# A one-core attention and mixer kernel: two fewer filler matmuls, the `u4` loads on another queue, and one semaphore step in place of two

## The chip, the cores and the metric

The kernel runs on one core of a Trainium2 chip. Its time is the device time of one execution in microseconds (us). It has five engines: TensorE (PE, with its weight loads shown apart as PEld), VectorE (DVE), ScalarE (ACT), GpSimd (POOL) and SyncE (SP), which issues DMAs.

## The reference

Attention with random features over 4 batches of 8 heads, 576 tokens and head size 64, then two mixers over the tokens and the channels:

```
def phi(x):                      # x: 576 x 64 of one head
    proj = x @ w_phi             # 128 features
    proj = proj - max(abs(proj)) # a maximum for each token
    return concat(exp(proj), exp(-proj))
kv, z = phi(k).T @ v, sum of phi(k) over the tokens
x = (phi(q) @ kv) / (phi(q) @ z + 1e-6)

u = x + (x.T @ U @ V).T          # U: 576 x 32, V: 32 x 576
x = u + relu(u @ w_ch1) @ w_ch2  # 512 -> 2048 -> 512
u = x + (relu(x.T @ w_tok1) @ w_tok2).T   # 576 -> 256 -> 576
out = u + relu(u @ w_ch1') @ w_ch2'       # 512 -> 1536 -> 512
```

## The kernel before

All products are taken in a short float format (fp32r) with a high and a low part: `a*b` is `a_hi*b_hi + a_hi*b_lo + a_lo*b_hi`, so that most matmuls come in threes. Heads are counted through: head `n` is head `n % 8` of batch `n // 8`. Two heads make a pair, `pn = n // 2`, since 2 times 64 channels fill the 128 partitions.

The program has three stages. In the **prologue** the 8 heads of batch 0 go through attention. In **block 1** PE works through the channel mixer in chunks of up to 512 tokens; woven into its matmuls, at places that tables of numbers give (`HEAD_STEPS`, `PAIR_STEPS`, `LAST_PAIR_STEPS`), are the attention steps of the 24 heads of batches 1 to 3. **Block 2** is the second mixer. Each engine has one instruction stream that runs in the order in which it is written, and waits on semaphores where its data come from another engine. Within a stream nothing overtakes a waiting instruction, but for weight loads.

Steps of one head: `proj_k` and `proj_qt` multiply the raw k and q (split into high and low part by `prep_k` and `prep_q` on ACT and POOL) by `w_phi`. `turn_r` turns q's block maxima on PE for the subtraction in `less_max`, `exp_k` and ACT's part of `less_max` take exponentials, `kv` builds the key-value product and `out` the head's output.

Three places matter here.

**The fillers.** `run_on_ones(count)` issues matmuls of ones whose result nobody reads. Each is two passes in the trace (a pass is one MATMUL record with its weight load). `WARM = 10, 5`: 10 at the start, and 5 ahead of `turn_r` of head 0, which waits for DVE's block maxima of q (`rq_done`).

**The loads of `u4`** (`U` of the first mixer, four copies side by side, 240 KB in six DMAs, whose contiguous pieces are 128 or 256 bytes of each partition and tile). They are issued from ACT's queue, two ahead of `kv` 0, two ahead of `exp_k` 1 and two ahead of `kv` 1. The first reader is PE's `pair_u` of head 1, which waits for all six (`u4_in`). SP's queue issues everything else that the prologue needs: for n = 2 to 8 the k of head n, its tail once more, the q of head n, the v of head n-1, and then one or two pieces of the mixer's weights (`load_w`). Some of these wait until POOL or PE has done with the buffer.

**The pairs.** For each of the 12 pairs of batches 1 to 3, PE turns the pair's output into token order (`pair_t`, L783), 5 tiles in the bank `ps_a`; ACT copies them, rounded, into XPH (`x_pair_hi`, L962 and L963). DVE then takes the remainders in two subtractions: L1157 for the first 4 tiles (into XPL, `x_pair_lo`), and L1159 for the fifth, which is only 64 tokens long and whose remainder is put on the upper 64 partitions of XPH's own fifth tile. Each subtraction raises `xl_done` by one. PE multiplies the high part by U in `pair_u` (L801, four matmuls) and the rest in `pair_l` (L808, five matmuls), with `less_max` of the next head (L727, two matmuls) between them for three pairs of four, and nothing between them for the last pair of a batch. `pair_l` waits for the first subtraction ahead of its first matmul and for the second ahead of its fifth.

Of the kernel before, what the change touches and what calls it, by code (L numbers as in the profile page):

```python
# [4 lines left out]
F32 = mybir.dt.float32  # L5
# [4 lines left out]
P = 128  # L10
B, H, S, DH = 4, 8, 576, 64
# [19 lines left out]
NB = S // TB  # L31
TURN = 72
WCH = 2 * D
WARM = 10, 5

K0 = 2 * P

# [292 lines left out]
def mixer_kernel(nc, k_t, q_t, v_aug, w_phi, u4, v4, mask_in, ident_in, wa, wb, wt1_in, wt2_in, x2_d, out):  # L330
# [181 lines left out]
    def wait(eng, name, value):  # L512
        if value > 0:
            eng.wait_ge(sem[name], value)
# [34 lines left out]
    def _(sp):  # L549
# [34 lines left out]
        for n in range(2, H + 1):  # L584
            load_k(n)
            load_k_again(n)
            load_q(n)
            load_v(n - 1)
            for i in ((n - 2,) if n < 6 else (2 * n - 8, 2 * n - 7)):
                load_w(i)  # L590
        load_v(H)
        for i in range(2 * H - 6, 4 * G1):
            load_w(i)
# [58 lines left out]
    def _(pe):  # L652
# [5 lines left out]
        def ring_free(use):  # L658
            if use >= AFTER:
                if use < AFTER + WIDE - RING:  # L660
                    pe.wait_ge(sem["x_done"], B * H)
                    pe.wait_ge(sem["xt_copied"], B * DT)
                    pe.wait_ge(sem["xl_done"], 2 * (B - 1) * DT)
                    pe.wait_ge(sem["kvl_done"], (B - 1) * H)
                    pe.wait_ge(sem["xu_lo"], B * DT)
                pe.wait_ge(sem["ring_read"], use - WIDE + 1)
            elif use >= RING:
                pe.wait_ge(sem["ring_read"], use - RING + 1)
            elif use < 2:
                pe.wait_ge(sem["qp_done"], 2 * (H - 1))  # L670
            else:
                pe.wait_ge(sem["x_done"], H)

        def turned_read(pairs):
            wait(pe, "xt_copied", pairs)
            wait(pe, "xl_done", 2 * (pairs - DT))

        def step(name, n, first=False):
            pn = n // 2
# [75 lines left out]
            elif name == "out":  # L755
                wait(pe, "tsum_done", 2 * (before(("proj_k",), (name, n)) - H) - 1)
                turned_read(before(("pair_t",), (name, n)))
                wait(pe, "x_done", n)
                wait(pe, "qp_done", 2 * n + 2)
                wait(pe, "kvl_done", steady(n))  # L760
                for a in range(2):
                    for c in range(2):
                        cols = slice(c * CW, (c + 1) * CW)
                        pe.matmul(x_ps[:, c, :], KVH[:, a, :], QPH[:, a, cols], start=(a == 0), stop=False)  # L764
                        pe.matmul(x_ps[:, c, :], KVL[:, a, :], QPH[:, a, cols], start=False, stop=False)  # L765
                for a in range(2):
                    pe.wait_ge(sem["qpl_done"], 2 * steady(n) - 1 + a)
                    for c in range(2):
                        cols = slice(c * CW, (c + 1) * CW)
                        last = pe.matmul(x_ps[:, c, :], KVH[:, a, :], QPL[:, a, cols], start=False, stop=(a == 1))  # L770
                last.then_inc(sem["out_done"], 1)
            elif name == "pair_t" and first:
                wait(pe, "x_done", n + 1)
                wait(pe, "diff_done", before(("proj_k",), (name, n)))
                for t in range(ST):
                    last = pe.transpose(xt_banks[:, t * P:(t + 1) * P], XP[:, t, :], ID[:])
                last.then_inc(sem["xt_done"], 1)
            elif name == "pair_t":
                wait(pe, "x_done", n + 1)
                wait(pe, "tsum_done", 2 * (before(("proj_k",), (name, n)) - H) - 1)  # L780
                for t in range(ST):
                    k = min(P, S - t * P)
                    last = pe.transpose(xt_banks[0:k, t * P:(t + 1) * P], UT[:, pn % DT, t * P:t * P + k], ID[:])  # L783
                last.then_inc(sem["xt_done"], 1)
            elif name == "pair_u":
                if first:
                    wait(pe, "x_done", n + 1)
                    wait(pe, "kv_copied", before(("kv",), (name, n)))
                    if n == 1:
                        pe.wait_ge(sem["u4_in"], loaded(6))  # L790
                    for t in range(ST):
                        last = pe.matmul(xu_bank(n), U4[:, t, :], XP[:, t, :], start=(t == 0), stop=(t == ST - 1))
                    last.then_inc(sem["xu_done"], 1)
                else:
                    wait(pe, "xt_copied", pn + 1)
                    wait(pe, "kvl_done", before(("kv",), (name, n)) - H)
                    wait(pe, "tsum_done", 2 * (before(("proj_k",), (name, n)) - H))
                    if pn == DT:
                        pe.wait_ge(sem["u_split"], 2)
                    for t in range(FULL):  # L800
                        pe.matmul(xu_bank(n)[0:2 * RANK], U2[:, t, 0:2 * RANK], XPH[:, t, :], start=(t == 0), stop=False)  # L801
            elif name == "pair_l":
                pe.wait_ge(sem["xl_done"], 2 * (pn - DT) + 1)
                for t in range(ST):
                    if t == FULL:
                        pe.wait_ge(sem["xl_done"], 2 * (pn - DT) + 2)
                    x = XPL[:, t] if t < FULL else XPH[:, FULL]
                    last = pe.matmul(xu_bank(n)[0:2 * RANK], U2[:, t, 0:2 * RANK], x, start=False, stop=(t == ST - 1))  # L808
                last.then_inc(sem["xu_done"], 1)
# [97 lines left out]
    def _(act):  # L907
# [90 lines left out]

        act.dma_start(WPR[0:DH, :], w_phi).then_inc(sem["wphi_in"], 16)
        act.dma_start(RAW[0:DH, S:SP], k_t[0, 0][:, FULL * P:S]).then_inc(sem["rk_again_0"], 16)  # L1000
        def load_u4(rows, tiles, source):
            for cols in (slice(0, RANK), slice(2 * RANK, P)):
                act.dma_start(U4[rows, tiles, cols], u4[source, tiles, cols]).then_inc(sem["u4_in"], 16)

        for name, n in PROLOGUE["act"]:
            if (name, n) == ("kv", 0):
                load_u4(slice(0, P), slice(0, FULL), slice(0, P))
            if (name, n) == ("exp_k", 1):
                load_u4(HALF[0], FULL, HALF[0])
            if (name, n) == ("kv", 1):  # L1010
                load_u4(HALF[1], FULL, HALF[0])
            if (name, n) == ("prep_q", 1):
                act.wait_ge(sem["ident_in"], loaded(1))
                act.copy(SPREAD[0:TB], ID[0:TB, 0:NB]).then_inc(sem["spread"], 1)
# [54 lines left out]
    def _(dve):  # L1069
        def step(name, n, first=False):  # L1070
# [83 lines left out]
            elif name == "pair_t" and not first:  # L1154
                dve.wait_ge(sem["kp_done"], 2 * before_on_dve(("proj_k",), (name, n)))
                dve.wait_ge(sem["xt_copied"], pn + 1)
                dve.tensor_tensor(XPL[:, 0:FULL].rearrange("p t f -> p (t f)"), xt_banks[:, 0:FULL * P],  # L1157
                                  XPH[:, 0:FULL].rearrange("p t f -> p (t f)").bitcast(F32), ALU.subtract).then_inc(sem["xl_done"], 1)
                dve.tensor_tensor(XPH[HALF[1], FULL], xt_banks[0:S_LAST, FULL * P:], XPH[0:S_LAST, FULL].bitcast(F32),  # L1159
                                  ALU.subtract).then_inc(sem["xl_done"], 1)  # L1160
            elif name == "pair_u":
# [259 lines left out]
```

## Time and profile before

| | us |
|---|---|
| median of 3 runs | 959.62 (959.57 to 959.8) |
| the profiled execution | 959.57 |
| its span, first to last instruction | 957.6 |
| PE busy in it | 953.1 |
| DVE, ACT, POOL busy | 510.1, 373.7, 238.1 |

What lies around the span, 959.57 - 957.6, is 2.0 us. Times within a trace are given as us from the span's start. Busy time of PE is the union of its records; a matmul's record is longer than the distance to the next one, since matmuls are pipelined.

### The profile page before, as it was taken

The page shows a single profiled execution, that of the slowest core. Times are in us where ns is not written, and L with a number is a line of the kernel's source. Part 1 is how long each engine was busy: PE and PEld are TensorE (multiplying, and loading weights), DVE is VectorE, ACT ScalarE, POOL GpSimd, SP SyncE. Part 2 cuts the span into 40 slices and gives each one's busy share as a digit, 9 for nine tenths or more (in the row PEclk, how much of TensorE's full clock was granted, in tenths as well). Part 3 has the DMA queues.
Part 4 walks back from the last instruction along what each step waited for, and adds up shares of the span by engine and source line. Part 5 has one row for each costly group of instructions (what it writes and reads, how often), then busy time and mean ns, then how long its engine had stood idle before and what let it go on. Part 6 is the DMA issues. An engine that isn't in the chain of part 4 may idle for free.

```text
span 957.6 us, 14160 instructions
## 1 busy us (share of the span) xinstructions
PE 953.1 (100%) x5402; PEld 830.3 (87%) x5402; DVE 510.1 (53%) x1005; ACT 373.7 (39%) x795; POOL 238.1 (25%) x148
## 2 busy tenths in 40 slices
PE   9999999999999999999999999999999999999998
PEld 8998888888888888888888889988888888888898
DVE  6756777667777658778543333433443343343232
ACT  6757667626665445665321112321212211111111
POOL 4357566704344214442120003430000000000000
PEclk9999999999999999999999999999999999999999
DMA  7661111111111021110052005542142132010010
GB/s 197 178 205 29 45 31 36 44 44 44 33 35 44 22 66 26 41 44 9 18 178 83 23 1 176 182 111 65 50 116 83 50 94 94 12 44 1 1 44 23
DMA packets 43042, 62.75 MB, mean 66 GB/s; under 512 B 10656, under 2 KB 30304, under 8 KB 41952
## 3 DMA queue, kind: packets, MB, share of 16 engines
q1 hardware_dynamic: 33376, 52.35, 18.7%
q10 hardware_dynamic: 9600, 9.50, 3.1%
q8 instruction: 44, 0.72, 0.3%
q14 instruction: 22, 0.18, 0.1%
HBM read 47.68 MB, written 14.16 MB: 65 GB/s over the span
## 4 chain that ended last, share of the span: by engine, by line
PE 98%; DVE 1%; DMA 0%; ACT 0%; issue 0%; ACTq 0%; DVEq 0%
PE ps_ring L872 50%; PE ps_a L872 15%; PE ps_m L872 8%; PE ps_m L743 6%; PE ps_ring L752 2%; PE ps_t L714 2%; PE ps_a L770 1%; PE ps_a L765 1%; PE ps_a L764 1%; PE ps_a L705 1%; PE ps_t L727 1%; PE ps_a L695 1%; PE ps_m L738 1%; PE ps_t L654 1%; PE ps_t L656 1%; PE ps_t L655 1%
## 5 line engine op out<-in xcount | busy, mean ns | idle before, releaser
L872 PE MATMUL ps_ring<-u_hi,w_hi 128*128 128x512 f32 (+1 forms) x376 | 143.6, 382 | 0.1
L872 PE MATMUL ps_ring<-h_hi,w_hi 128*128 128x512 f32 (+1 forms) x376 | 143.0, 380 | 0.1
L872 PE MATMUL ps_ring<-u_hi,w_lo 128*128 128x512 f32 (+1 forms) x376 | 141.1, 375 | 0.0
L872 PE MATMUL ps_ring<-u_lo,w_hi 128*128 128x512 f32 (+1 forms) x376 | 141.0, 375 | 0.0
L872 PE MATMUL ps_ring<-h_lo,w_hi 128*128 128x512 f32 (+1 forms) x376 | 140.8, 374 | 0.0
L872 PE MATMUL ps_ring<-h_hi,w_lo 128*128 128x512 f32 (+1 forms) x376 | 140.6, 374 | 0.0
L1035 ACT ACTIVATE h_hi<-ps_ring 128x512 fp32r<-128x512 f32 (+1 forms) x94 | 53.1, 565 | 174.2 <-PE ps_ring L872 173.4
L1262 DVE SCALAR_TENSOR_TENSOR h_lo<-ps_ring,h_hi 128x512 fp32r<-128x512 f32 (+1 forms) x94 | 60.8, 648 | 106.1 <-ACT h_hi L1035 105.9
L1327 POOL TENSOR_TENSOR q_features_lo<-q_features_t,q_features_hi 128x576 fp32r<-128x576 f32 x48 | 67.8, 1433 | 115.7 <-ACT q_features_t L954 115.7
L1345 POOL TENSOR_TENSOR w_lo<-w_raw,w_hi 128x1024 fp32r<-128x1024 f32 x28 | 67.5, 2427 | 116.5 <-ACT w_hi L985 115.3
L872 PEld LDWEIGHTS ps_ring<-h_lo,w_hi 128*128 128x128 f32 x376 | 70.8, 188 | 13.3 <-DVE h_lo L1262 0.2
L872 PEld LDWEIGHTS ps_ring<-u_hi,w_lo 128*128 128x128 f32 x376 | 70.8, 188 | 13.2
L872 PEld LDWEIGHTS ps_ring<-u_hi,w_hi 128*128 128x128 f32 x376 | 70.9, 189 | 12.0 <-DVE h_lo L1262 0.5
L872 PEld LDWEIGHTS ps_ring<-h_hi,w_hi 128*128 128x128 f32 x376 | 71.0, 189 | 11.2 <-DVE acc L1197 0.5
L872 PEld LDWEIGHTS ps_ring<-u_lo,w_hi 128*128 128x128 f32 x376 | 71.0, 189 | 9.6
L872 PEld LDWEIGHTS ps_ring<-h_hi,w_lo 128*128 128x128 f32 x376 | 71.0, 189 | 9.4
L1197 DVE TENSOR_TENSOR acc<-ps_ring,acc 128x512 f32<-128x512 f32 (+1 forms) x67 | 43.3, 647 | 56.9 <-PE ps_ring L872 56.6
L1338 POOL TENSOR_TENSOR q_split<-kq_raw,q_split 64x640 fp32r<-64x640 f32 x27 | 41.8, 1550 | 62.0 <-ACT q_split L923 54.8
L1333 POOL TENSOR_TENSOR k_split<-kq_raw,k_split 64x640 fp32r<-64x640 f32 x27 | 42.2, 1563 | 57.2 <-ACT k_split L919 52.7
L743 PE MATMUL ps_m<-v_one,k_features 128*128 128x66 f32 x448 | 53.1, 272 | 0.0
L743 PEld LDWEIGHTS ps_m<-v_one,k_features 128*128 128x128 f32 x448 | 52.2, 192 | 0.0
L1035 ACT ACTIVATE h_hi<-ps_a 128x512 fp32r<-128x512 f32 (+1 forms) x30 | 15.8, 526 | 84.5 <-PE ps_a L872 84.0
(218 smaller groups left out, 1951.2 us busy)
## 6 DMA issues: line engine op xcount, KB each, us to landing
w_raw<-in_wa SPq DMA_DIRECT2D x16, 512.0 KB, 5.1
w_raw<-in_wb SPq DMA_DIRECT2D x12, 512.0 KB, 4.2
v_one<-in_v_aug SPq DMA_DIRECT2D x28, 165.0 KB, 2.2
x_features<-x_scratch SPq DMA_DIRECT2D x4, 1152.0 KB, 6.1
x_by_tokens<-x_turned SPq DMA_DIRECT2D x16, 288.0 KB, 5.3
u_full<-x_scratch SPq DMA_DIRECT2D x4, 1152.0 KB, 5.2
kq_raw<-in_q_t SPq DMA_DIRECT2D x28, 160.0 KB, 2.9
x_tokens<-x_by_tokens SPq DMA_DIRECT2D x16, 256.0 KB, 2.7
```

Source lines behind the costliest of these rows:

```text
L654: pe.matmul(ps, wh, xh, start=first, stop=False)
L714: last = pe.matmul(turned_ps(n)[:, c, :], WP[:, i, :], sq(n)[:, c * CW:(c + 1) * CW], start=(i == 0), stop=(i == 1))
L743: last = pe.matmul(kv_ps[:, a, :], kp(n)[:, 2 * t + a], v(n)[:, t, :], start=False, stop=(a == 1 and t == FULL - 1))
L752: last = pe.matmul(out_bank[0:k, t, :], QP[:, a, t * P:t * P + k], KV[:, a, 0:VC], start=(a == 0), stop=(a == 1))
L872: last = pe.matmul(ps, w, x, start=(k, m) == (0, 0), stop=ended)
L1035: act.activation(HH[:, j, 0:n], bank(use, n), ACT.Relu).then_inc(sem["h_hi"], 1)
L1197: dve.tensor_tensor(ACC[:, j, 0:n], ps, ACC[:, j, 0:n], ALU.add).then_inc(sem["ring_read"], 1)
L1262: dve.scalar_tensor_tensor(out=HL[:, j, 0:n], in0=bank(USE[block_no, c, u], n), scalar=0.0, in1=HH[:, j, 0:n].bitcast(F32), op0=ALU.max, o ...
L1327: pool.tensor_tensor(QPL[:, a, 0:S], QP[:, a, 0:S], QPH[:, a, :].bitcast(F32), ALU.subtract).then_inc(sem["qpl_done"], 1)
L1333: pool.tensor_tensor(sk(n)[DH:P, :], raw_kq(n)[0:DH, :], sk(n)[0:DH, :].bitcast(F32), ALU.subtract).then_inc(sem["k_split_lo"], 1)
L1338: pool.tensor_tensor(sq(n)[0:DH, :], raw_kq(n)[DH:P, :], sq(n)[DH:P, :].bitcast(F32), ALU.subtract).then_inc(sem["q_split_lo"], 1)
L1345: pool.tensor_tensor(WL[place], WR[place], WH[place].bitcast(F32), ALU.subtract).then_inc(sem["w_lo"], 1)
```

## The change

It has three parts. Two of the five fillers ahead of `turn_r` 0 go. The six `u4` loads leave ACT's queue and are issued from SP's, one after another, behind the first piece of the mixer's weights and ahead of the k of head 3; their shapes are the same, their order differs a little. And `xl_done` is raised once for a pair, by the second subtraction, so that all five matmuls of `pair_l` come after one wait for it; the counts of the other waits on `xl_done` are halved to match.

```diff
-WARM = 10, 5
+WARM = 10, 3
...
             for i in ((n - 2,) if n < 6 else (2 * n - 8, 2 * n - 7)):
                 load_w(i)
+            if n == 2:
+                for cols in (slice(0, RANK), slice(2 * RANK, P)):
+                    sp.dma_start(U4[:, 0:FULL, cols], u4[:, 0:FULL, cols]).then_inc(sem["u4_in"], 16)
+                    for rows in HALF:
+                        sp.dma_start(U4[rows, FULL, cols], u4[HALF[0], FULL, cols]).then_inc(sem["u4_in"], 16)
...
-                    pe.wait_ge(sem["xl_done"], 2 * (B - 1) * DT)
+                    pe.wait_ge(sem["xl_done"], (B - 1) * DT)
...
-            wait(pe, "xl_done", 2 * (pairs - DT))
+            wait(pe, "xl_done", pairs - DT)
...
-                pe.wait_ge(sem["xl_done"], 2 * (pn - DT) + 1)
+                pe.wait_ge(sem["xl_done"], pn - DT + 1)
                 for t in range(ST):
-                    if t == FULL:
-                        pe.wait_ge(sem["xl_done"], 2 * (pn - DT) + 2)
...
-        def load_u4(rows, tiles, source):
-            for cols in (slice(0, RANK), slice(2 * RANK, P)):
-                act.dma_start(U4[rows, tiles, cols], u4[source, tiles, cols]).then_inc(sem["u4_in"], 16)
-
         for name, n in PROLOGUE["act"]:
-            if (name, n) == ("kv", 0):
-                load_u4(slice(0, P), slice(0, FULL), slice(0, P))
-            if (name, n) == ("exp_k", 1):
-                load_u4(HALF[0], FULL, HALF[0])
-            if (name, n) == ("kv", 1):
-                load_u4(HALF[1], FULL, HALF[0])
...
                 dve.tensor_tensor(XPL[:, 0:FULL].rearrange("p t f -> p (t f)"), xt_banks[:, 0:FULL * P],
-                                  XPH[:, 0:FULL].rearrange("p t f -> p (t f)").bitcast(F32), ALU.subtract).then_inc(sem["xl_done"], 1)
+                                  XPH[:, 0:FULL].rearrange("p t f -> p (t f)").bitcast(F32), ALU.subtract)
```

On PE, the end of a pair in block 1, with each row's waits. Before:

```order
L727 MATMUL ps_t<-q_max_rows,minus_ones 128x288
L808 MATMUL ps_m<-x_pair_lo,u_split 64x128 [waits xl_done]
L808 MATMUL ps_m<-x_pair_lo,u_split 64x128 x3
L808 MATMUL ps_m<-x_pair_hi,u_split 64x128 [waits xl_done]
L872 MATMUL ps_ring<-h_hi,w_hi 128x512 [waits h_hi,w_lo,ring_read]
```

and after the change, with the new line numbers:

```order
L732 MATMUL ps_t<-q_max_rows,minus_ones 128x288
L811 MATMUL ps_m<-x_pair_lo,u_split 64x128 [waits xl_done]
L811 MATMUL ps_m<-x_pair_lo,u_split 64x128 x3
L811 MATMUL ps_m<-x_pair_hi,u_split 64x128
L875 MATMUL ps_ring<-h_hi,w_hi 128x512 [waits h_hi,w_lo,ring_read]
```

No matmul moves; the fifth one's wait is gone, and the first one's now stands for both subtractions.

On SP's queue, between the first piece of weights and the k of head 3 (`u_82` is `u4`):

```order
@@ -14,4 +14,8 @@
 L568 DMA v_one_odd<-in_v_aug 64x66
 L574 DMA w_raw<-in_wa 128x1024
+L593 DMA u_82<-in_u 128x4x32
+L595 DMA u_82<-in_u 64x32 x2
+L593 DMA u_82<-in_u 128x4x64
+L595 DMA u_82<-in_u 64x64 x2
 L553 DMA kq_raw_odd<-in_k_t 64x576
 L557 DMA kq_raw_odd<-in_k_t 64x64
```

Six DMAs are put in; all that stood behind them keeps its order.

## Rows read from the trace of the kernel before

**Rows 1.** The page: busy us of each engine; PE's granted clock in 40 slices.
```profile
PE 953.1 (100%) x5402; PEld 830.3 (87%) x5402; DVE 510.1 (53%) x1005; ACT 373.7 (39%) x795; POOL 238.1 (25%) x148
...
PEclk9999999999999999999999999999999999999999
```

**Rows 2.** Waits of PE: us in total, times, longest us.
```profile
PE ps_t L727 <- DVE q_max_rows L1119: 0.2, 1, 0.2
```

**Rows 3.** Timeline, an ordinary pair: start us, us, engine, line, count.
```profile
114.45 0.69 DVE L1157 TENSOR_TENSOR x_pair_lo<-ps_a,x_pair_hi 128x512 fp32r<-128x512 f32 x1 [0.44 <-ACT x_pair_hi L963]
...
115.03 0.48 PE L727 MATMUL ps_t<-q_max_rows,minus_ones 128*128 128x288 f32 x2
115.17 0.28 DVE L1159 TENSOR_TENSOR x_pair_hi<-ps_a,x_pair_hi 64x128 fp32r<-64x128 f32 x1
...
115.35 0.40 PE L808 MATMUL ps_m<-x_pair_lo,u_split 128*64 128x128 f32 x4
...
115.59 0.23 PE L808 MATMUL ps_m<-x_pair_hi,u_split 128*64 128x128 f32 x1
...
115.65 0.44 PE L872 MATMUL ps_ring<-h_hi,w_hi 128*128 128x512 f32 x1
```

**Rows 4.** Timeline, the last pair of a batch.
```profile
198.33 0.28 DVE L1159 TENSOR_TENSOR x_pair_hi<-ps_a,x_pair_hi 64x128 fp32r<-64x128 f32 x1
...
198.36 0.45 PE L808 MATMUL ps_m<-x_pair_lo,u_split 128*64 128x128 f32 x4
198.67 0.27 PE L808 MATMUL ps_m<-x_pair_hi,u_split 128*64 128x128 f32 x1
198.78 0.45 PE L872 MATMUL ps_ring<-h_hi,w_hi 128*128 128x512 f32 x1
```

**Rows 5.** Line L1159: count, ns min/median/max, first and last start us.
```profile
L1159 DVE TENSOR_TENSOR x_pair_hi<-ps_a,x_pair_hi x12: 283/283/285, 115.2 to 467.2; 64x128 fp32r<-64x128 f32 x12
```

**Rows 6.** Timeline of DVE, two neighbours that each raise a semaphore.
```profile
78.15 1.23 DVE L1097 TENSOR_REDUCE k_proj_sum<-ps_a 128x512 f32<-128x1024 f32 x1 [0.34 <-PE ps_m L705]
79.29 0.41 DVE L1098 TENSOR_REDUCE k_proj_sum<-ps_m 128x128 f32<-128x256 f32 x1
```

**Rows 7.** Timeline of PE at the start: the fillers and `turn_r` 0.
```profile
1.00 4.53 PE L879 MATMUL ps_m<-k_features_odd 128*64 128x128 f32 x20 [1.00 <-POOL k_features_odd L1310]
...
7.84 1.31 PE L879 MATMUL ps_m<-k_features_odd 128*64 128x128 f32 x10
9.53 0.28 PE L722 MATMUL ps_ring<-ident,q_block_max 128*72 128x128 f32 x1 [0.39 <-DVE q_block_max L1106]
```

**Rows 8.** Timeline of SP's queue: issues of the first weights, k 3, q 3, v 3.
```profile
8.98 0.59 SPq L574 DMA_DIRECT2D w_raw<-in_wa  x1
9.80 0.47 SPq L553 DMA_DIRECT2D kq_raw_odd<-in_k_t  x1
...
11.41 0.47 SPq L562 DMA_DIRECT2D kq_raw_odd<-in_q_t  x1
...
18.43 0.33 SPq L567 DMA_DIRECT2D v_one_odd<-in_v_aug  x1
```

**Rows 9.** Tile `u`: the issues on ACT's queue, ns min/median/max.
```profile
L1003 ACTq DMA_DIRECT2D u<-in_u x6: 389/516/837, 11.1 to 16.5; - x6
```

**Rows 10.** Timeline of ACT: the splits of q 3 and k 3, `kv` 1, `less_max` 1.
```profile
16.60 0.72 ACT L923 CAST q_split_odd<-kq_raw_odd 64x640 fp32r<-64x640 f32 x1
17.35 0.72 ACT L919 CAST k_split_odd<-kq_raw_odd 64x640 fp32r<-64x640 f32 x1
18.43 0.27 ACT L944 COPY v_k<-ps_m 128x132 f32<-128x132 f32 x1 [0.36 <-PE ps_m L743]
19.19 1.19 ACT L954 ACTIVATE q_features_t<-ps_t 128x576 f32<-128x576 f32 x2 [0.48 <-PE ps_t L727]
```

**Rows 11.** DMA issues, KB each, us to landing: q 3's alone, and the page's median.
```profile
kq_raw_odd<-in_q_t SPq DMA_DIRECT2D x1, 160.0 KB, 4.5
```
```profile
kq_raw<-in_q_t SPq DMA_DIRECT2D x28, 160.0 KB, 2.9
```

## Prediction, written before the run

> **What bounds the kernel now.** I read the page first, for which engine has no idle time; then the waits of PE, for whether anything makes it wait; then the timelines of the three places that the change touches, row by row, because none of them is large enough to show in a sum.
>
> The page says that PE is busy for 953.1 of 957.6 us and DVE for 510.1 [rows 1]. So PE is the bound, and not on average only: among the waits that the trace lists, the only one of PE behind the first 10 us is 0.2 us for DVE's `q_max_rows` [rows 2]. It follows that **every tenth that PE loses anywhere is lost at the end**, and that what other engines gain is worth nothing unless PE waits for it. But the list has a blind spot. Two matmuls that start a little late because of a semaphore still look busy, since a record is longer than the step to the next. One has to look at the distances between starts, and that is where the largest term of this change lies.
>
> **Part 1, the pairs (12 times).** Nothing is taken from PE's work. What changes is what its first of five matmuls waits for: the second subtraction (L1159) rather than the first (L1157). There are 12 such places, all alike [rows 5].
>
> *Ordinary pair (9 of 12)* [rows 3]. The first subtraction ends at 114.45 + 0.69 = 115.14. PE starts the first of the five at 115.35, behind `less_max`, the fifth at 115.59 and the mixer's next matmul at 115.65. The second subtraction ends at 115.17 + 0.28 = 115.45. So before the change, PE began the four matmuls while DVE was still at the fifth tile, and the fifth came just when that was ready. Afterwards all five start behind 115.45.
>
> How long from DVE's end to PE's start? The last pair of a batch shows that [rows 4]: L1159 ends at 198.33 + 0.28 = 198.61, the matmul that waits for it starts at 198.67, 0.06 later. And what do five matmuls take from a standing start? There too: the group of four has records that last 0.45 together, against 0.40 in a running stream [rows 3], so standing costs 0.05 more. In the running stream the fifth follows the first by 115.59 - 115.35 = 0.24; from a standing start I take 0.24 + 0.05 = 0.29 to 0.30.
>
> Ordinary pair after the change: start at 115.45 + 0.06 = 115.51, fifth at 115.51 + 0.30 = 115.81, next matmul one step of 0.06 later, 115.87, against 115.65: **+0.22**.
>
> *Last pair of a batch (3 of 12)* [rows 4]. The fifth is held by the second subtraction already, at 198.67, and the next matmul follows at 198.78. After: first at 198.67, fifth at 198.97, next at 199.03: **+0.25**.
>
> Sum: 9 x 0.22 + 3 x 0.25 = 1.98 + 0.75 = **2.7 us**. Behind it no work is idle enough to give this back: PE is in no debt to anyone that a later slack could repay [rows 1, 2], and each of the others gets its input from PE later by the same amount. Bounds: at the low end the standing start costs nothing (fifth 0.24 behind the first), 9 x 0.16 + 3 x 0.19 = 2.0; at the high end each place costs what the fifth was ahead of in a last pair, the whole of 198.67 - 198.36 = 0.31, so 12 x 0.31 = 3.7.
>
> The missing step of the semaphore might help DVE: would L1159 start earlier if L1157 raised nothing? L1159 starts 0.03 behind L1157's end [rows 3]. The neighbours L1097 and L1098 do overlap: 78.15 + 1.23 = 79.38, but L1098 starts at 79.29, 0.09 before, and L1097 does raise a semaphore [rows 6]. So raising one is not what keeps L1159 back, and taking it away should not let it go earlier. I put 0 here; as a rival it is priced below.
>
> The Trainium skill has a rule on just this (VectorE: DVE Perf Modes, "Two Vector instructions with no wait between them"): an instruction whose output starts in another group of 32 partitions than the last output is held until all earlier ones are done, and a semaphore operation plays no part in it. L1159 writes the upper half where L1157 wrote from partition 0. By that rule part 1 costs the 2.7 us; without it, were L1159 free to overlap, it would be the 1.4 us of the first rival.
>
> **Part 2, the fillers.** The five fillers are ten records in 1.31 us, from 7.84 to 9.15; `turn_r` 0 starts at 9.53, released by DVE after PE had been idle for 0.39 [rows 7]. Two fewer are four records, 4 x 0.131 = 0.52 us, which only lengthen that idle time to some 0.9 us. Time saved: 0, since DVE's block maxima are what is late. The fillers hide nothing but the quiet of PE, and what that quiet may cost is its clock. The granted clock reads full in every slice [rows 1], but the pace of the fillers tells more: 4.53 / 20 = 0.227 us a record for the first ones, 0.131 for the later ones [rows 7], so the first ran at 1.2 GHz and the later ones at 2.4. A fall back would double the duration of what follows. I take 0, because PE is quiet for 0.4 us already without any slowing behind it, and 0.9 is closer to that than to nothing at all having run; the other end is in the rivals.
>
> **Part 3, the `u4` loads.** ACT loses six issues of 0.39 to 0.84 us [rows 9]. They are issued by its sequencer beside running work, and ACT's steps around them are released by PE [rows 10]: no gain. SP gets them between the end of the first weights' issue, 8.98 + 0.59 = 9.57, and k 3 [rows 8]. At six times the median of 0.52 that is 3.1, with small gaps 3.3 us: k 3 is issued at about 12.9 rather than 9.80, q 3 some 1.1 us later, at 14.0 rather than 11.41. Behind them v 2, the next weights, k 4 and q 4 move too, by less and less, until v 3, which waits for PE until 18.43 in any case [rows 8]; from there on SP is as before.
>
> Who misses k 3 and q 3? ACT, in order: it splits q 3 at 16.60, k 3 at 17.35, then copies `kv` 1 and takes `less_max` 1 at 19.19, for which PE waits [rows 10]. From the start of q 3's split to the earliest `less_max` it is 0.75 + 0.75 + 0.30 = 1.8 us, so q 3 may land as late as 19.19 - 1.8 = 17.4 at no cost. Landing took 4.5 us there, in a stretch crowded by weights, and 2.9 in the median [rows 11]. The two ends are 14.0 + 2.9 = 16.9, cost 0, and 14.0 + 4.5 = 18.5, cost 18.5 - 17.4 = 1.1 us of PE. In between: before, q 3 landed at 11.41 + 4.5 = 15.9 with much of `u4` still on its way, and now all of `u4` goes ahead of it in the same queue. Its 240 KB are 1.5 times q 3's 160 KB, in small pieces; a delay of 1.5 us or so gives 17.4, right at the edge. I take **0.1 us**.
>
> **Sum.** 2.7 + 0 + 0.1 = 2.8 us. The profiled execution would take 959.57 + 2.8 = 962.4 (a span of 957.6 + 2.8 = 960.4), and since it lies 0.05 from the median of 959.62, the median too: **962.4 us**.
>
> **Rivals.**
>
> *DVE starts its second subtraction earlier (not slower).* One mechanism at one place: if it is the raised semaphore after all that separates L1157 and L1159, then L1159 moves from 0.03 behind to 0.08 or 0.09 before L1157's end, as L1098 does [rows 6], 0.11 earlier. If the five matmuls also cost nothing extra from a standing start, a pair costs 0.16 - 0.11 = 0.05 and a last pair 0.19 - 0.11 = 0.08, in all 0.7 us; with the extra, 9 x 0.11 + 3 x 0.14 = 1.4 us, and 0.1 for part 3. The time is 960.3 to 961.1, of which I take 961.0, close to the end that keeps the extra. It decides from 0.16 us a pair downwards: 12 x 0.16 is the 1.9 us below which a measurement would call it no change. For it: both instructions work on different tiles and nothing in the code makes the second wait. Against: the pair in [rows 6] overlaps with its semaphore.
>
> *The pairs cost nothing.* The starts of modelled records are not exact, and the first four matmuls may already come so late in truth that the fifth's wait is the same wait. Then the time is 959.6 to 960.0. Against it: all 12 places read alike [rows 5], and starts, unlike ends, are recorded.
>
> *ACT misses q 3.* The upper end of part 3, 1.1 us of PE lost near 19, on top of the 2.7: 959.6 + 2.7 + 1.1 = 963.4. For it: that stretch of SP's queue is full.
>
> *PE's clock falls in the longer quiet ahead of `turn_r` 0.* Then the PE work behind 9.53 runs at half pace for some us; each us of it costs another, 2 to 3 us at the rate of the first fillers [rows 7]. Time: 964.4 to 965.4. Against it: the remaining fillers still stand ahead of it.
>
> *Faster.* It would take a gain that no row offers: the fillers and ACT's issues are both in time that nobody waits for. I leave 0.02 for a mechanism that I can't name.
>
> **How the numbers follow.** Chances: the forecast (a loss of 2.0 to 3.4 us) 0.70; DVE earlier 0.11; no cost 0.06; ACT misses q 3 0.08; clock 0.03; faster 0.02. A measurement of this kernel tells a change from none at about 0.2%, 1.9 us, so slower begins at 961.5. Slower: 0.70 + 0.08 + 0.03, less a little for forecasts at their low end, 0.80. Within 0.2%: 0.11 + 0.06 + that little, 0.18. Faster: 0.02. The range goes down to the first rival's time, 961.0, and up to 963.9, over the upper bound of part 1 (959.6 + 3.7 + 0.1 = 963.4) and the third rival. What is left out is no cost, the clock, faster, and the lower half of the first rival, some 0.16.
>
> **What would show it.** In the timeline after the change, in each of the 12 places all five matmuls of `pair_l` start behind the end of the second subtraction, the first 0.06 later; the mixer's next matmul follows the second subtraction's end by 0.42 (115.87 - 115.45) rather than 0.20. If that distance is 0.3, the standing start is cheap; if the second subtraction starts before the first one ends, the first rival holds. The trace's waits of PE should now list this line, which they did not. For part 3: k 3 issued at about 12.9, and `less_max` 1 on ACT at 19.2 if the slack held. For part 2: `turn_r` 0 at 9.53 as before, and then the same pace. I would be wrong above all if the distances between starts in [rows 3, 4] are an artefact, since all of 2.7 us rests on them.

## The result, and the profile after

The change makes the kernel slower: 966.29 us in the median of four executions (965.09 to 968.15), against 959.66 for the kernel before on the same chip (959.57 to 959.8). The ratio is 1.007, with an interval of 1.0051 to 1.009. The prediction was 962.4 us with a range of 961.0 to 963.9: right in its sign, too low by 3.9 us, and the time lies above the range.

The profiled execution of the changed kernel took 961.59 us (span 959.6), which would have fitted the forecast. It is not typical, and that is the first finding. Its granted clock was 1.000; the four others had spans of 963.0 to 966.1 us and mean granted clocks of 0.995 to 0.996. A mean of 0.996 over 963.0 us means 0.004 x 963.0 = 3.9 us of clock missing, 0.995 over 966.1 us means 4.8; the third digit is rounded, so each is good to 0.5. The kernel before had 1.000 in every execution whose clock is listed. So two questions stand: where did the 2.0 us of the profiled execution go, and what takes PE's clock in the others?

The waits of PE after the change, where before there was one entry behind the first 10 us [rows 2] (engine, tile and line that wait, the releaser; us in total, times, longest us):

```profile
PE ps_ring L727 <- DVE q_block_max L1099: 0.8, 1, 0.8
PE ps_m L743 <- ACT k_features L938: 0.7, 1, 0.7
PE ps_m L811 <- DVE x_pair_hi L1152: 0.6, 3, 0.3
...
PE ps_t L732 <- DVE q_max_rows L1112: 0.2, 1, 0.2
```

The third is the pairs, which the prediction asked for. The first is the quiet that the missing fillers leave, also foreseen. The second is new, and the prediction has nothing on it: PE's `kv` 2 waits for ACT's `k_features`. Of the twelve pairs this list of PE shows three. The list of the weight loads (PEld) shows all of them:

```profile
PEld ps_m L811 <- DVE x_pair_hi L1152: 3.0, 12, 0.4
```

**The pairs.** Timeline of the changed kernel, all engines, the ordinary pair that answers to [rows 3] (start us, us, engine, line, count):

```profile
115.14 0.69 DVE L1150 TENSOR_TENSOR x_pair_lo<-ps_a,x_pair_hi 128x512 fp32r<-128x512 f32 x1 [0.44 <-ACT x_pair_hi L966]
...
115.84 0.28 DVE L1152 TENSOR_TENSOR x_pair_hi<-ps_a,x_pair_hi 64x128 fp32r<-64x128 f32 x1
...
116.18 0.46 PE L811 MATMUL ps_m<-x_pair_lo,u_split 128*64 128x128 f32 x4
...
116.48 0.22 PE L811 MATMUL ps_m<-x_pair_hi,u_split 128*64 128x128 f32 x1
...
116.54 0.44 PE L875 MATMUL ps_ring<-h_hi,w_hi 128*128 128x512 f32 x1
```

DVE ends at 115.84 + 0.28 = 116.12, the first matmul starts 0.06 behind it, the fifth 0.30 behind the first, and the mixer 0.06 behind the fifth: 0.42 from DVE's end to the mixer, as forecast, against 0.20 before.

**The start.** Timeline of PE (the last number in square brackets is its idle time before the row, and who ended it):

```profile
7.68 0.87 PE L882 MATMUL ps_m<-k_features_odd 128*64 128x128 f32 x6
9.38 0.28 PE L727 MATMUL ps_ring<-ident,q_block_max 128*72 128x128 f32 x1 [0.84 <-DVE q_block_max L1099]
```

The three fillers end at 7.68 + 0.87 = 8.55 and `turn_r` 0 follows when DVE has its maxima. This whole trace lies 0.15 us earlier than that of before [rows 7], and PE had been idle for 0.84 instead of 0.39.

**The loads.** Timeline of the changed kernel, SP's queue, ACT and PE, which answers to [rows 8] and [rows 10]:

```profile
9.46 0.44 SPq L593 DMA_DIRECT2D u<-in_u  x1
...
11.78 1.15 SPq L595 DMA_DIRECT2D u<-in_u  x2
...
12.98 0.60 SPq L553 DMA_DIRECT2D kq_raw_odd<-in_k_t  x1
...
14.27 0.59 SPq L562 DMA_DIRECT2D kq_raw_odd<-in_q_t  x1
...
17.19 1.64 SPq L557 DMA_DIRECT2D kq_raw<-in_k_t  x1
17.34 0.72 ACT L926 CAST q_split_odd<-kq_raw_odd 64x640 fp32r<-64x640 f32 x1 [0.91 <-DMA kq_raw_odd<-in_q_t]
...
19.04 1.19 ACT L957 ACTIVATE q_features_t<-ps_t 128x576 f32<-128x576 f32 x2
...
22.01 0.72 ACT L922 CAST k_split<-kq_raw 64x640 fp32r<-64x640 f32 x1 [1.78 <-DMA kq_raw<-in_k_t]
...
23.70 0.46 PE L743 MATMUL ps_m<-v_one,k_features 128*128 128x132 f32 x2 [0.70 <-ACT k_features L938]
```

And the same view of the kernel before, of the stretch that the prediction did not look at:

```profile
14.40 0.60 SPq L557 DMA_DIRECT2D kq_raw<-in_k_t  x1
...
20.30 0.73 ACT L919 CAST k_split<-kq_raw 64x640 fp32r<-64x640 f32 x1
...
21.97 0.40 ACT L929 ACTIVATE k_features<-k_proj_less_max_first,sign 128x128 f32<-128x128 f32 x1 [0.95 <-DVE k_proj_less_max_first L1090]
...
23.04 0.46 PE L738 MATMUL ps_m<-v_one,k_features 128*128 128x132 f32 x2
```

Read the two together. k 3 and q 3 move as forecast (12.98 and 14.27 for a forecast of 12.9 and 14.0), ACT takes `less_max` 1 at 19.04: q 3 costs nothing. But behind them k 4 moves by nearly as much: its second piece is issued at 17.19 rather than 14.40. ACT splits k 4 just ahead of the exponentials of `exp_k` 2, in order. Before, that split started at 20.30 and could have started 0.95 later, since `exp_k` 2 waited that long for DVE. Now the data lets ACT start only at 22.01, `exp_k` 2 follows, and PE starts `kv` 2 at 23.70 instead of 23.04.

The account of the profiled execution: at the mixer's first matmul, at 62.27 before and 62.93 after, the changed kernel is 0.66 us behind; the twelve pairs add 0.17 to 0.24 each, some 2.4; about 1.1 of that is given back in between (the fourth experiment shows where); it ends 2.02 behind.

### The profile page after: what moved, and what is told of

It is laid out like the page before. It is cut to its first block, busy times and chain, and to the rows that moved or that the text cites. A ratio compares the mean times of both kernels' runs of the same rounds, so it can differ in the third digit from the quotient of the medians.

```text
span 959.6 us, 14152 instructions
## 1 busy us (share of the span) xinstructions
PE 953.0 (99%) x5398; PEld 828.7 (86%) x5398; DVE 510.3 (53%) x1005; ACT 373.4 (39%) x795; POOL 238.1 (25%) x148
## 4 chain that ended last, share of the span: by engine, by line
PE 97%; SPq 1%; DMA 1%; DVE 1%; issue 0%; ACT 0%; ACTq 0%; DVEq 0%
PE ps_ring L875 50%; PE ps_a L875 15%; PE ps_m L875 8%; PE ps_m L748 5%; PE ps_t L719 2%; PE ps_ring L757 1%; PE ps_a L775 1%; PE ps_a L770 1%; PE ps_a L769 1%; PE ps_a L710 1%; PE ps_t L732 1%; PE ps_t L661 1%; PE ps_t L660 1%; PE ps_t L659 1%; PE ps_m L743 1%; PE ps_a L788 1%
```

## The experiments

All are the kernel before with one edit, except the fifth and the last. "Before" was timed beside each, at 959.59 to 959.85 us.

**1. Three fillers instead of five.**

```
-WARM = 10, 5
+WARM = 10, 3
```

> The kernel before with WARM = 10, 3 and nothing else. Theory A (the two fillers cost the clock): most executions 963 to 966 us, with a mean granted clock of 0.995 to 0.996 in them, while an execution that happens to keep full clock takes 959.5. Theory B (the clock is lost only where several longer quiet stretches of PE come together, so not by the fillers alone): 959.6, clock 1.000 throughout. Theory C (the clock has nothing to do with the fillers): 959.6 as well.

Measured: 959.61 us (959.21 to 960.0, 10 executions), ratio 0.9998, interval 0.9989 to 1.0008, the clock 1.000 in all. Part 2 costs nothing, though PE waits 0.8 us for `turn_r` 0.

**2. No fillers ahead of `turn_r` 0.**

```
-WARM = 10, 5
+WARM = 10, 0
```

> The kernel before with WARM = 10, 0, so that PE is quiet for about 1.7 us ahead of turn_r 0. Theory A: at least as slow as with 3 fillers, 963 to 968, and the profile should show where the clock is low: matmul steps of 0.11 us twice as far apart in the stretch behind 9.5 us, or the slow pace of the first fillers lasting longer. Theories B and C: 959.6, since nothing waits for the fillers.

Measured: 974.68 us (974.39 to 975.05, 4 executions), ratio 1.0153, interval 1.0138 to 1.0168, the clock 0.982 in all. In its trace PE is idle for 1.9 us ahead of `turn_r` 0, where with five fillers it was 0.39. Its windows (stretch us; busy time of PE, PEld, DVE, ACT and POOL with counts; PE's granted clock; DMA share; GB/s):

```profile
8.00:10.00 2.00, 0.45 (x2) 0.35 (x3) 1.41 (x2) 1.25 (x3) 1.93 (x2) 0.83 0.91 275
10.00:12.00 2.00, 2.00 (x11) 2.00 (x11) 1.41 (x4) 0.81 (x2) 1.93 (x2) 0.50 0.84 219
...
42.00:44.00 2.00, 2.00 (x14) 2.00 (x14) 0.85 (x3) 0.80 (x3) 0.39 (x1) 0.63 0.05 6
44.00:46.00 2.00, 2.00 (x20) 1.86 (x20) 1.29 (x3) 1.53 (x3) 0.37 (x1) 1.00 0.04 12
```

The clock falls to 0.50, its lower level of 1.2 GHz, in the quiet ahead of `turn_r` 0, and stays there for some 34 us (9.3 to 43.5) although PE is busy all the time: 11 matmuls in 2 us where there were 19. The fillers do hold the clock, and a fall costs far more than the quiet that brings it.

**3. The `u4` loads alone.** The six issues stand on SP where the change puts them; the rest is as before.

```
+            if n == 2:
+                for cols in (slice(0, RANK), slice(2 * RANK, P)):
+                    sp.dma_start(U4[:, 0:FULL, cols], u4[:, 0:FULL, cols]).then_inc(sem["u4_in"], 16)
...
-            if (name, n) == ("kv", 0):
-                load_u4(slice(0, P), slice(0, FULL), slice(0, P))
...
```

> The kernel before with only the u4 loads moved to SP's queue ahead of k 3. From the profile of the changed kernel: exp_k 2 on ACT comes late behind the split of k 4, PE waits 0.7 us at kv 2, in all +0.6 to +0.8: 960.3, clock 1.000. If the extra 0.7 us of quiet is what costs the clock (theory B or C): above 963 in most executions.

Measured: 965.22 us (963.64 to 965.84, 4 executions), ratio 1.0053, interval 1.0036 to 1.007, clocks of 0.994 to 0.996. So the part that was costed at 0.1 us brings most of the loss. Its profiled execution (964.74 us) fell into the typical case. The wait of PE:

```profile
PE ps_m L743 <- ACT k_features L940: 1.5, 1, 1.5
```

And its windows:

```profile
22.00:24.00 2.00, 1.52 (x14) 1.19 (x12) 1.41 (x4) 0.67 (x2) 0.16 (x1) 1.00 1.05 300
24.00:26.00 2.00, 0.97 (x9) 1.01 (x10) 1.75 (x6) 1.40 (x4) 1.54 (x1) 1.00 0.55 118
26.00:28.00 2.00, 2.00 (x16) 2.00 (x16) 0.00 (x0) 0.48 (x2) 0.00 (x0) 0.79 0.01 3
28.00:30.00 2.00, 2.00 (x11) 2.00 (x11) 0.18 (x1) 1.12 (x3) 0.00 (x0) 0.50 0.75 150
...
32.00:34.00 2.00, 2.00 (x12) 2.00 (x11) 0.85 (x3) 0.98 (x3) 0.20 (x1) 0.51 0.17 33
34.00:36.00 2.00, 2.00 (x19) 1.86 (x19) 0.96 (x3) 1.34 (x3) 0.56 (x1) 1.00 0.00 0
```

Here is the mechanism. PE, busy without a gap from 20 on, is quiet between 23.5 and 25.0 because `kv` 2 waits. Behind that the clock goes to half, from about 27.1 to 34, and PE works through that stretch at 11 matmuls in 2 us. The missing clock is, window by window, 2 x 0.21 + 2 x 0.50 + 2 x 0.50 + 2 x 0.49 = 3.4 us. `kv` 2 itself started at 25.02, which is 2.0 later than before. Together that is 5.4, and the execution is 964.74 - 959.57 = 5.2 longer.

In the changed kernel's own profile the wait was shorter, 0.70, and the clock held:

```profile
22.00:24.00 2.00, 1.29 (x12) 1.00 (x11) 1.34 (x5) 1.99 (x4) 1.24 (x2) 1.00 0.78 266
24.00:26.00 2.00, 2.00 (x20) 2.00 (x19) 1.29 (x4) 0.14 (x2) 0.34 (x1) 1.00 0.62 142
```

**4. The pairs alone.** One raise of `xl_done` behind the second subtraction, as in the change.

```
-                pe.wait_ge(sem["xl_done"], 2 * (pn - DT) + 1)
+                pe.wait_ge(sem["xl_done"], pn - DT + 1)
                 for t in range(ST):
-                    if t == FULL:
-                        pe.wait_ge(sem["xl_done"], 2 * (pn - DT) + 2)
...
```

> The kernel before with only the one xl_done step per pair. By the steps in the trace of the changed kernel: 12 places of +0.20 = +2.4, of which about 1.1 comes back at short waits of PE further on that the delay hides, so +1.3: 960.9 to 961.0. By the prediction as written (nothing comes back): 962.3. If the clock were lost here: above 963.

Measured: 961.11 us (960.48 to 962.13, 10 executions), ratio 1.0012, interval 1.0003 to 1.0022: 1.4 us, half of the 2.7 forecast. In its trace, as in that of the whole change, each of the 12 pairs puts PE back by about 0.2, and some 1.1 us comes back between them, a little at a time. Two places show how, in the kernel before and in the whole change. The first is the loads of `proj_k`'s weights, before and after (PEld: start us, us, count, idle before):

```profile
173.75 0.53 PEld L705 LDWEIGHTS ps_a<-w_phi_split,k_split 128*128 128x128 f32 x4 [0.37 <-issue]
```
```profile
174.84 0.53 PEld L710 LDWEIGHTS ps_a<-w_phi_split,k_split 128*128 128x128 f32 x4 [0.20 <-issue]
```

PE is busy in both, yet the loader stood still for 0.37 before and stands for 0.20 now; the mixer's next matmul is 0.17 less late behind it. The second, before the change:

```profile
333.08 0.19 PEld L872 LDWEIGHTS ps_ring<-h_hi,w_hi 128*128 128x128 f32 x1 [0.51 <-DVE acc L1197]
```

and the same load after the change:

```profile
334.72 0.19 PEld L875 LDWEIGHTS ps_ring<-h_hi,w_hi 128*128 128x128 f32 x1 [0.27 <-DVE acc L1190]
```

This load waits for DVE's `acc` both times, but for 0.27 instead of 0.51: the matmul ahead of it is 1.87 late, the load itself 1.64, and 0.24 come back. Most of these stops are at the loads for `proj_k`, of which the list of waits of the kernel before says:

```profile
PEld ps_a L705 <- issue: 2.4, 9, 0.4
```

After the change it is 1.9 for the same nine. That these short stops are slack is shown by the difference of the starts; what ends those that read `issue` was not tested.

**5. The whole change with five fillers.**

```
-WARM = 10, 3
+WARM = 10, 5
```

> The whole change, but with WARM = 10, 5 as before. Theory D (the loss is the late k 4, which makes PE wait at kv 2 and then costs it the clock, plus the pairs; the fillers do nothing): 965 to 967, clock 0.995 to 0.996, as the whole change. If the missing fillers lengthen or bring on the slow clock when the other parts are there: back to about 961.6, clock 1.000.

Measured: 966.82 us in the median of six executions, ratio 1.0063, interval 1.0043 to 1.0083 (both without the longest one). One had a clock of 1.000 and took 961.9; four took 965.23 to 968.3 at 0.995 and 0.996; one took 978.45 at 0.983. The two fillers make no difference to the whole change either. The profiled one (967.6 us) has the wait at `kv` 2 at 1.9 us and the clock at 0.50 from 25.4 to 35.7, which is 5.1 us of missing clock. It is the only trace of the three parts together in which the clock fell: `kv` 2 starts at 25.00, 2.0 later than before, and 2.0 + 5.1 + 1.4 for the pairs is 8.5, for a measured 965.6 - 957.6 = 8.0 of span. The four slower executions of the changed kernel itself have no trace; that their clock fell at the same place is concluded from this one and the third experiment.

**6. Six tiny DMAs on SP, `u4` still on ACT.** Each brings 32 bytes a partition into a tile that nobody reads.

```
+            if n == 2:
+                for j in range(6):
+                    sp.dma_start(TINY[:, 8 * j:8 * j + 8], mask_in).then_inc(sem["tiny_in"], 16)
```

> The kernel before, u4 still loaded from ACT's queue, and in addition six tiny DMAs (128 x 8 numbers each, into a tile nobody reads) on SP's queue at the place where the change puts the u4 loads. Theory D1 (what delays k 4 is that SP is kept busy issuing, some 3.3 us): PE waits 0.7 to 1.5 us at kv 2, 964 to 966 with a clock below 1. Theory D2 (it is the u4 bytes in small pieces, ahead of k 3 to k 4 in one queue): 959.6 to 960.0, clock 1.000.

Measured: 960.32 us (959.94 to 966.06, 10 executions), ratio 1.0015, interval 1.0 to 1.0029. Eight lie at 959.94 to 960.78 with the clock at 1.000; two took 964.21 and 966.06, at 0.996 and 0.995. The profiled one, of the first kind:

```profile
9.52 3.04 SPq L594 DMA_DIRECT2D tiny<-in_mask  x6
...
16.18 0.47 SPq L554 DMA_DIRECT2D kq_raw<-in_k_t  x1
...
22.14 0.72 ACT L923 CAST k_split<-kq_raw 64x640 fp32r<-64x640 f32 x1 [1.26 <-DMA kq_raw<-in_k_t]
```

The 3.0 us of issuing by themselves bring k 4's split from 20.30 to 22.14 and `kv` 2 from 23.04 to 23.83, with a wait of PE of 0.2 there. In the whole change the split was at 22.01, in the third experiment at 23.33. So against the third experiment SP's issue time is the larger part of the delay, 1.8 of 3.0 us. Where the clock fell in the two slower executions no trace shows. The fall is usual in the third experiment and rare here, so the rest of the delay matters too. That this rest comes from the bytes of `u4` ahead of k 4 is argued and not shown: the profiled execution of the whole change has those bytes, and its split is no later than here.

**7. The `u4` loads on SP, behind q 4.** The same six issues with `if n == 4`, between `load_q(4)` and `load_v(3)`.

```
             load_q(n)
+            if n == 4:
+                for cols in (slice(0, RANK), slice(2 * RANK, P)):
...
             load_v(n - 1)
```

> The kernel before with only the u4 loads moved to SP's queue, but behind q 4, ahead of v 3, where SP waits for PE in any case. Theory D: k 4 and q 4 are untouched, so no wait at kv 2; SP is some 1 us late afterwards and v 3 has slack: 959.6, clock 1.000. If moving the u4 loads off ACT's queue is itself what costs (their bytes, or their landing before pair_u of head 1): over 962.

Measured: 959.58 us (959.27 to 960.11, 10 executions), ratio 0.9999, interval 0.9989 to 1.0008, the clock 1.000 in all. The move from ACT to SP by itself costs nothing; what costs is the place of the loads, ahead of k 3 and k 4.

**8. Two fillers.**

```
-WARM = 10, 5
+WARM = 10, 2
```

> The kernel before with WARM = 10, 2: PE is quiet for about 1.1 us ahead of turn_r 0. With 3 fillers and 0.8 us nothing was lost, with none and 1.55 us the clock was low from 9 to 43 us. If the length of that quiet decides step by step: about 959.6 in most executions, a few at 965 or more. If the number of fillers hardly matters until the last are gone: 959.6 throughout.

Measured: seven of ten executions took 959.37 to 960.92 us at 1.000, three 972.96 to 973.23 at 0.984; median 959.96, ratio 1.0043, interval 1.0001 to 1.0084. The profiled one is of the first kind, and the fall did not come in it, though PE waited longer than with three fillers:

```profile
PE ps_ring L722 <- DVE q_block_max L1106: 1.2, 1, 1.2
```

So the same program, at the same place, keeps its clock in one execution and loses it in another.

**9. The third experiment with twenty fillers ahead of `kv` 2.** This separates the quiet from the lateness, since k 4 is as late as before.

```
                 wait(pe, f"v_in_{n % 2}", loaded(2 * (n // 2 + 1)))
+                if n == 2:
+                    WPS = WP[:, 0]
+                    for _ in range(20):
+                        pe.matmul(ps_m[:, 0:DF], WPS, WPS, start=True, stop=True)
```

> The kernel before, with the six u4 loads on SP at n == 2 as in e3_u4_sp, and 20 filler matmuls (128x128, some 0.06 us each, 1.2 us) on PE ahead of kv 2, between its wait for v and its wait for the k features. They fill most of the quiet that the late k 4 makes there (1.5 us in e3_u4_sp) and take nothing away from its lateness. Theory A (the lateness costs PE some 1 to 2 us, and the rest of e3_u4_sp's 5.5 us is PE's clock, which falls because PE is quiet at that place): the granted clock is 1.000 in all executions, and the time 960.6 to 961.8 us. Theory B (the clock falls for something else that the move does near 20 to 26 us, the transfers for instance, whatever PE does there): the clock is .994 to .996 as in e3_u4_sp and the time 964 to 966. Theory C (the lateness itself costs PE more than the wait shows, and the clock is a small part): clock 1.000, time 963 or more.

Measured: 961.61 us (961.37 to 962.59, 9 executions), ratio 1.0023, interval 1.0012 to 1.0033; the clock is 1.000 in eight and 0.998 in one. Timeline of PE and ACT, and the windows:

```profile
22.96 2.43 PE L745 MATMUL ps_m<-w_phi_split 128*128 128x128 f32 x20
23.09 0.73 ACT L928 CAST k_split<-kq_raw 64x640 fp32r<-64x640 f32 x1 [2.64 <-DMA kq_raw<-in_k_t]
...
25.23 0.44 PE L747 MATMUL ps_m<-v_one,k_features 128*128 128x132 f32 x2
```
```profile
24.00:26.00 2.00, 2.00 (x20) 2.00 (x20) 1.50 (x4) 1.16 (x3) 1.45 (x1) 1.00 0.95 245
26.00:28.00 2.00, 2.00 (x20) 2.00 (x19) 0.00 (x0) 0.51 (x2) 0.00 (x0) 1.00 0.07 19
```

`kv` 2 starts at 25.23, 2.2 later than before and even 0.2 later than in the third experiment, the same loads are issued in the same order, and yet the kernel is 3.6 us faster than that one, 961.61 against 965.22, because PE was not quiet. The 2.0 us that remain over before are the lateness of `kv` 2. Theory A holds, and B and C fall. (The fillers took 0.12 us each, not the 0.06 expected, and so were a little too long: they, and no longer the features, release `kv` 2. By the 0.75 us from the start of ACT's exponentials over 128x512 (24.27) to `kv` 2 in the third experiment, here 24.03 + 0.75 = 24.8, they hold it for about 0.4 us, an estimate.)

**10. The whole change with the `u4` loads behind q 4.**

```
-            if n == 2:
+            if n == 4:
```

(with the block moved up between `load_q(n)` and `load_v(n - 1)`, as in the seventh).

> The whole change, but with the u4 loads on SP behind q 4 (n == 4) rather than ahead of k 3, as in e7_u4_late. Theory A (of the change's 6.6 us the place of the u4 loads is all but the pairs' part, and the fillers are nothing): the pairs' 1.4 us alone are left, 960.8 to 961.4, clock 1.000, and no wait of PE at kv 2. Theory D (the three parts add up to more than each alone, for instance since fewer fillers and a later start of the pairs together leave PE more quiet near its limits): 963 or more, or a clock below 1 in several executions.

Measured: 961.13 us in the median. Nine of ten executions took 960.66 to 962.57 at 1.000, one took 974.8 at 0.984; ratio 1.0032, interval 1.0004 to 1.006. The median is 1.5 over before: the pairs' part and nothing else. The one outlier has the clock and the time of the outliers of the eighth experiment. Such a long fall came in none of the ten executions with three fillers alone, but it may also be what the 978.45 us of the fifth experiment are, with a clock of 0.983 and all five fillers. So it is rare rather than tied to the two fillers, and what brings it is open.

No version came out faster than the kernel before by more than the noise: each of the three parts costs something or nothing.

## Why the prediction was wrong, step by step

**What bounds the kernel: right.** "Every tenth that PE loses anywhere is lost at the end" held for `kv` 2, with one exception below.

**Part 1, the pairs: the mechanism right, its sum twice too large.** The distances came out as worked out: 0.06 from DVE to PE, 0.30 over the five matmuls, 0.17 to 0.24 a pair. The rival of an earlier second subtraction fell: it starts 0.70 behind the first (115.84 - 115.14), against 0.72 before [rows 3]. That is 0.02 nearer, at all twelve places, and not the 0.11 of the rival, and nothing overlaps. By the Trainium skill's rule that the prediction quoted (VectorE: DVE Perf Modes, "Two Vector instructions with no wait between them") the second subtraction is held with or without a semaphore, and the trace agrees with its 0.70. The step that failed is "behind it no work is idle enough to give this back". It was read off the list of waits, in which PE matmuls that keep busy have none; yet the weight loads in front of them stand still for up to 0.51 us at some places (the list of PEld's waits has nine stops of up to 0.4 at `proj_k` alone), and a PE that comes late there catches up. The 12 delays of about 0.20, some 2.4 in all, become 1.4 us, as the fourth experiment has it, instead of 2.7. The prediction itself had warned that this list has a blind spot, and applied that to the loss only.

**Part 2, the fillers: right.** Zero, by the first and the fifth experiment. The rival that the clock falls there was real as a mechanism (second and eighth experiments, with fewer fillers than the change leaves) but was sized wrongly: it gave 2 to 3 us of loss for a fall that takes 13 to 15, since the half clock lasts for some 34 us (second) rather than "some us". Its reading of the first fillers' pace holds: in the trace of the fourth experiment ten filler records at a granted clock of 0.50 take 2.40 us, 0.24 each, so 0.227 each at the start is near the lower level, though the view lists 1.00 there.

**Part 3, the `u4` loads: this is where the prediction failed.** The term "I take 0.1 us" measured 5.5 us by itself (third experiment, 965.22 against 959.72). The prediction looked at q 3, found the slack held at the edge, and wrote that k 4 and q 4 "move too, by less and less, until v 3". k 4's second piece moved by 2.8 us (14.40 to 17.19), not less than k 3's first by much (3.2). Who needs k 4 was never asked. The method that it used for q 3 would have shown the danger: k 4's split at 20.30 had 0.95 of slack, and the landings of the kernel before between 9 and 20 us list its second piece (KB, us to landing):

```profile
kq_raw<-in_k_t SPq DMA_DIRECT2D x1, 16.0 KB, 5.6
```

With the issue time measured after the change, 17.19 + 5.6 = 22.8 against 20.30 + 0.95 = 21.25: 1.5 us late. The runs show `kv` 2 late by 0.7 (whole change, profiled), 2.0 (third, and fifth) and 2.2 (ninth, some 0.4 of it from its fillers).

On the same step the Trainium skill says (DMA: Bandwidth & Descriptors, "Issuing engines are not separate DMA queues") that issuing from several engines saves only the sequencer's time to start a DMA, usually small beside the DMA. Here the six issues took 3.5 us in a row on SP (9.46 to 12.93), and in the sixth experiment 3.0 us of issuing alone put k 4's split back by 1.8: in a queue whose next entries are due, that time is not small.

**The clock: a rival at the wrong place.** It stood ahead of `turn_r` 0 with a chance of 0.03. The place is `kv` 2, where before the change PE had no quiet at all. The prediction costed a wait at its own length; a wait in this part of the kernel costs its length and, in most executions, the half clock behind it, 3.4 us in the third experiment and 5.1 in the fifth. That this part, 3.5 of the third experiment's 5.5 us, comes from PE's quiet, and not from the transfers or the lateness, is what the ninth experiment shows.

**The sum, corrected.** Missing clock is the most that a fall can cost, since some of it lies beside other waits (second experiment: 34 us at half are 17 missing, for a loss of 15.0). Pairs 1.4, lateness of `kv` 2 0.7 to 2.0, clock 3.9 to 4.8: 6.0 to 8.2 over 959.66, so 965.7 to 967.9, for a measured 965.09 to 968.15. The profiled execution is 1.36 + 0.66 = 2.02, without the clock.

**What stays open.** Why k 4 lands at different times in equal programs (its split is at 22.01 in the whole change, 23.31 in the fifth experiment); in most of the traces, that of the kernel before too (1.40), one of SP's issues takes 1.3 to 2.0 us instead of some 0.5, at different entries, and in the changed kernel and the ninth experiment it was k 4's own second piece (1.64 and 2.03); why was not tested. And where in the 978.45 us execution of the fifth experiment the clock fell.

## What to carry to other kernels

When DMAs are put into a queue, follow every later entry of it until the queue waits for something else, and ask of each who reads it and by when; the first reader's slack says nothing about the second's. Price a new wait of PE with the clock that it may cost, which can be more than the wait, and if it can't be avoided, try dummy matmuls in it. When a delay is added at many places of a PE-bound stream, look for short stops of the weight loads between them (the waits of PEld, not those of PE) before multiplying: they give part of it back.

## What the runs showed of the hardware

The half clock lasts very unequal times. After the quiet ahead of `turn_r` 0 it was 34 us with PE busy throughout (second experiment), after the quiet ahead of `kv` 2 some 7 and 10 us (third and fifth), and in the profiled execution of the fourth it came early, for some 3.4 us (7.7 to 11.1), with all five fillers in place:

```profile
4.00:6.00 2.00, 1.30 (x9) 0.91 (x7) 1.29 (x6) 1.17 (x3) 0.00 (x0) 1.00 0.73 187
6.00:8.00 2.00, 1.89 (x12) 1.72 (x13) 1.84 (x4) 1.90 (x5) 0.00 (x0) 0.92 0.40 99
8.00:10.00 2.00, 2.00 (x10) 1.72 (x9) 1.85 (x3) 1.20 (x3) 1.50 (x1) 0.50 0.96 301
10.00:12.00 2.00, 2.00 (x15) 1.67 (x14) 0.57 (x3) 1.30 (x3) 1.85 (x3) 0.73 0.87 204
```

Ahead of it PE stood still twice at `proj_k` 0, where the trace of the kernel before has no wait; the 20 fillers of the start took 3.97 us here instead of the 4.53 of [rows 7]:

```profile
5.48 0.33 PE L695 MATMUL ps_a<-w_phi_split,k_split 128*128 128x128 f32 x1 [0.51 <-DVE k_split L1073]
6.11 1.35 PE L695 MATMUL ps_a<-w_phi_split,k_split 128*128 128x128 f32 x9 [0.31 <-DVE w_phi_split L1077]
```

That fall cost 1.0 us against the median of its kernel (962.13 against 961.11) and shows that even this start can lose its clock without the change's quiet. Whether a given quiet costs the clock also differs from execution to execution of one program. Ahead of `turn_r` 0, with the quiet as the one profiled execution has it, the clock fell in none of ten with 0.8 us (three fillers), in three of ten with 1.2 (two) and in four of four with 1.9 (none); with the tiny DMAs in two of ten. A profile is one execution, and here it was one that most others did not resemble; the granted clock listed for each of them told so.
